# Heads of one parity form a quad: k, q and v are loaded over 128 partitions, w_in over 64

## The reference

```python
def _attn_ref(q, k, v, p):
    scale = 1.0 / np.sqrt(q.shape[-1])
    def sm_attn(qq, kk, vv):
        s = scale * np.matmul(qq, kk.transpose(0, 1, 3, 2))
        ...                      # softmax over the last axis, into a
        return np.matmul(a, vv)
    p_packed = sm_attn(p, k, v)
    return sm_attn(q, p_packed, p_packed)

def reference(...):
    x = attn_out.transpose(0, 2, 1, 3).reshape(4608, 512)
    h = x @ w_in                            # 512 -> 1024
    x = layernorm(h * softmax(h)) @ w_out   # 1024 -> 512
    h = max(x @ w1, x @ w2, x @ w3)         # 512 -> 768
    return h @ w_out2                       # 768 -> 512
```

## Time and profile before

| | |
|---|---|
| median of 3 runs | 1097.89 us |
| the profiled execution | 1094.8 us |
| its span, first to last instruction | 1093.2 us |
| TensorE busy in the span | 94% |
| VectorE, ScalarE, GpSimd busy | 55%, 32%, 23% |
| loads of k, q and v | 64 transfers, 28.3 MB of 183.2 MB moved |
| mean granted TensorE clock | 0.978 of full speed |

### The profile page before, as it was taken

One profiled execution on the slowest core, in us unless ns is written; L12 is line 12 of the kernel. 1 busy time (PEld: TensorE's weight loads), 2 busy tenths in 40 slices (PEclk: granted clock), 3 DMA queues, 4 the chain that ended last, 5 costly groups with the idle time before them and its releaser, 6 DMA issues.

```text
span 1093.2 us, 15814 instructions
## 1 busy us (share of the span) xinstructions
PE 1030.2 (94%) x6498; PEld 815.8 (75%) x6498; DVE 606.3 (55%) x980; ACT 345.6 (32%) x551; POOL 250.8 (23%) x222
## 2 busy tenths in 40 slices
PE   5778868799999999999999999999999999999998
PEld 4444534487888888888888888888888888888887
DVE  1367757767657747765646653667355563654021
ACT  3345544333423414432422233222322142222111
POOL 0112354448398439832000000000000000000000
PEclk9789989899999999999999999999999999999999
DMA  9988985234366145511575444554455535543251
GB/s 201 247 214 205 250 216 148 100 138 156 118 233 227 65 156 179 223 44 77 212 279 188 176 166 162 183 179 179 154 186 176 185 137 191 177 156 112 98 171 39
DMA packets 47144, 183.23 MB, mean 168 GB/s; under 512 B 8032, under 2 KB 8032, under 8 KB 37472
## 3 DMA queue, kind: packets, MB, share of 16 engines
q1 hardware_dynamic: 40848, 147.21, 42.6%
q0 software_dynamic: 6224, 35.00, 8.7%
HBM read 134.62 MB, written 47.58 MB: 167 GB/s over the span
## 4 chain that ended last, share of the span: by engine, by line
PE 78%; DVE 9%; DMA 5%; issue 4%; ACT 2%; POOL 1%; SPq 1%; ACTq 0%
PE ps L1088 27%; PE ps L723 24%; PE ps L1120 13%; PE ps L1111 4%; PE ps L737 2%; PE ps L988 2%; DMA q_raw<-in_q_dram 2%; PE ps L870 2%; DMA w_in_s<-in_moe_w_in_dram 2%; DVE a2T L1570 1%; DMA k_raw<-in_k_dram 1%; DVE h_lo L1479 1%; DVE spot L1776 1%; PE ps L828 1%; DVE spot L1767 1%
## 5 line engine op out<-in xcount | busy, mean ns | idle before, releaser
L1088 PE MATMUL ps<-ys,slot 128*128 128x512 f32 x1512 | 345.8, 390 | 0.5
L1088 PEld LDWEIGHTS ps<-ys,slot 128*128 128x128 f32 x1512 | 283.3, 188 | 62.4 <-ACT spot L1163 3.9
L1767 DVE TENSOR_TENSOR spot<-ps,spot 128x512 f32<-128x512 f32 x108 | 74.3, 688 | 99.7 <-PE ps L1088 74.2
L1163 ACT ACTIVATE spot<-ps 128x512 f32<-128x512 f32 x90 | 52.8, 596 | 207.5 <-PE ps L1088 196.4
L723 PE MATMUL ps<-ln_hi,w_out_s_lo 128*128 128x512 f32 x280 | 109.1, 390 | 0.0
L723 PE MATMUL ps<-ln_hi,w_out_s_hi 128*128 128x512 f32 x280 | 109.0, 389 | 0.0
L723 PE MATMUL ps<-ln_lo,w_out_s_hi 128*128 128x512 f32 x280 | 109.0, 389 | 0.0
L1120 PE MATMUL ps<-w_out_s_lo,h_hi 128*128 128x512 f32 x216 | 84.1, 389 | 0.0
L1120 PE MATMUL ps<-w_out_s_hi,h_lo 128*128 128x512 f32 x216 | 84.1, 389 | 0.0
L1120 PE MATMUL ps<-w_out_s_hi,h_hi 128*128 128x512 f32 x216 | 84.1, 389 | 0.0
L1294 ACT ACTIVATE u<-ps,neg_max 128x1024 f32<-128x1024 f32 x36 | 40.2, 1117 | 124.0 <-DVE neg_max L1645 124.0
(11 more groups left out here) (152 smaller groups left out, 1500.9 us busy)
## 6 DMA issues: line engine op xcount, KB each, us to landing
slot<-w_operands SPq DMA_DIRECT2D x36, 1792.0 KB, 7.3
w_operands<-stage POOLq DMA_DIRECT2D x18, 1024.0 KB, 4.9
k_raw<-in_k_dram SPq DMA_DIRECT2D x32, 288.0 KB, 5.9
v_raw<-in_v_dram SPq DMA_DIRECT2D x16, 576.0 KB, 9.4
q_raw<-in_q_dram SPq DMA_DIRECT2D x16, 576.0 KB
y_features<-yst SPq DMA_DIRECT2D x9, 1024.0 KB, 4.4
y_raw<-y_features SPq DMA_DIRECT2D x9, 1024.0 KB, 5.6
out_dram<-spot SPq DMA_DIRECT2D x36, 256.0 KB, 2.1
```

The source lines that it names most:

```text
L1088: last = pe.matmul(ps[:, group_bank(g, k), :], w[:, a - 1, i, kk, :], ys[:, b, j, kk, :], start=n < 4 and kk == 0 and e == 0, stop=kk == K ...
L1163: return act.activation(dst, src, ACT.Copy)
L1767: dve.tensor_tensor(dst[:, :], a, b, op).then_inc(ready, 1)
```

## The change

A quad is now the heads of one parity: quad g holds the heads g, g + 2, g + 4, g + 6. The view of k, q and v merges quad and partition: partition 64g + p reads at p x 2304 bytes behind the start of head g, which for one pair of heads is one run of neighbouring rows over all 128 partitions. So k comes in two transfers a batch (576 KB each), v and q in one each (1152 KB). The rows of w_in that belong to the heads of a quad are no longer 128 neighbours: `w_in_s` is filled by four transfers of 512 KB, each over 64 partitions and two blocks. `p` and its tile stay as they were; `scores1` picks other columns of the transposed p (`small`). The counts that TensorE waits for change with the number of transfers. Engine instructions are the same in number and shape.

```diff
-    w_in_v = w_in.rearrange("(k p) n -> p k n", p=P)
+    w_in_v = w_in.rearrange("(x l g d) n -> l d g x n", l=2, g=QUADS, d=D)
...
     def rows(t):
-        return t.rearrange("b (g h) (p j) d -> b g p h (j d)", g=QUADS, j=J)
+        return t.rearrange("b (h g) (p j) d -> b (g p) h (j d)", g=QUADS, j=J)
...
                 for x in range(2):
-                    for g in range(QUADS):
-                        sp.dma_start(k_raw[half(g), 2 * x:2 * x + 2, :, :].rearrange("p h j d -> p h (j d)"),
-                                     k_v[b, g][:, 2 * x:2 * x + 2, :]).then_inc(k_loaded[x], 16)
+                    at = slice(2 * x, 2 * x + 2)
+                    sp.dma_start(k_raw[:, at, :, :].rearrange("p h j d -> p h (j d)"), k_v[b][:, at, :])\
+                        .then_inc(k_loaded[x], 16)
...
-                for g in range(QUADS):
-                    sp.dma_start(v_raw[half(g), :, :, :].rearrange("p h j d -> p h (j d)"), v_v[b, g])\
-                        .then_inc(v_loaded, 16)
+                sp.dma_start(v_raw[:, :, :, :].rearrange("p h j d -> p h (j d)"), v_v[b]).then_inc(v_loaded, 16)
...
-                for g in range(QUADS):
-                    sp.dma_start(q_raw[half(g), :, :, :].rearrange("p h j d -> p h (j d)"), q_v[b, g])\
-                        .then_inc(q_loaded, 16)
+                sp.dma_start(q_raw[:, :, :, :].rearrange("p h j d -> p h (j d)"), q_v[b]).then_inc(q_loaded, 16)
...
                 if b == 0:
-                    sp.dma_start(w_in_s[:, :, :], w_in_v).then_inc(w_in_loaded, 16)
+                    for l in range(2):
+                        for g in range(QUADS):
+                            sp.dma_start(w_in_s[half(l), 2 * g:2 * g + 2, :], w_in_v[l][:, g]).then_inc(w_in_loaded, 16)
...
                 def small(jj, h):
-                    return pT[jj * D:(jj + 1) * D, g, h * NPACK:(h + 1) * NPACK]
+                    n = QUADS * h + g
+                    return pT[jj * D:(jj + 1) * D, n // QH, n % QH * NPACK:(n % QH + 1) * NPACK]
```

More of the change, by code:

```diff
@@ L761, in turn_k @@
                 if j % 2 == 0:
-                    pe.wait_ge(k_loaded[min(j // 2, 1)], 32 * b + 32)
+                    pe.wait_ge(k_loaded[min(j // 2, 1)], 16 * b + 16)
                 turn_rows(bank, k_raw, j).then_inc(kT_filled, 1)
@@ L815, in turn_q @@
                 if j == 0:
-                    pe.wait_ge(q_loaded, 32 * b + 32)
+                    pe.wait_ge(q_loaded, 16 * b + 16)
                 turn_rows(bank, q_raw, j).then_inc(qT_filled, 1)
             def pack(b):
-                pe.wait_ge(v_loaded, 32 * b + 32)
+                pe.wait_ge(v_loaded, 16 * b + 16)
                 pe.wait_ge(a1T_first, 2 * b + 2)
@@ L856, in merge @@
                 if b == 0:
-                    pe.wait_ge(w_in_loaded, 16)
+                    pe.wait_ge(w_in_loaded, 64)
                 if b == B - 1:
```

## The result

| | before | after |
|---|---|---|
| median | 1098.22 us (4 runs, 1094.13 to 1101.03) | 1079.72 us (4 runs, 1078.86 to 1080.79) |
| profiled execution | 1094.8 us | 1078.86 us |
| its span | 1093.2 us | 1077.1 us |

The ratio after to before is 0.9835, 95% interval 0.9802 to 0.9868: 18.5 us or 1.7% less by the medians, 15.9 us between the two profiled executions. The change is faster, by 1.3 to 2.0% in the interval.

What follows compares the result with a forecast made beforehand. TensorE was taken to bound the kernel at 78%, with most load time hidden; 3 + 0 + 3.5 + 1.5 + 0.8 + 2 = 10.8 us off gave 1084 from the profiled execution, 1087 from the median, said as 1085, 8-in-10 range 1073 to 1094.

Steps and rivals of the forecast that it cites:

- a wait for w_in above 4 us: Sign named beforehand: TensorE waiting longer than this for w_in in the profile after would show the prediction wrong.
- Step 1: Start of the kernel, first loads of k and those of batch 1: 3 us saved, bounds 1.5 to 4.
- Step 2: Load of w_in, needed at the merge of batch 0: no change, bounds -1.5 to +2 us.
- The rival "slower": At the merge of batch 0, w_in's four slices land so late that the gain is lost: 1100 us, chance 0.04.
- Step 3: Load of q for batch 5: 3.5 us less wait, bounds 1.8 and 4.2, and 1.5 us of clock behind it.
- Step 4: Load of q for batch 7: 0.8 us of TensorE's wait saved, bounds 0 and 1.8.
- Step 5: TensorE's "issue" waits in pack and scores2, read as code fetches partly queueing behind data: 2 us saved, bounds -1 and 8.
- The rival "more than the sum": Attention stage: fetches (8), w_in's wait (1.5) and clock (another 4) gain beyond the forecast: 1073 us, chance 0.17.

Runs made afterwards that it cites:

- The second experiment: The changed kernel with as many transfers of k, q and v as before, each over 128 partitions: 1081.17 us, ratio 0.9829 to the kernel before.
- the first: The changed kernel with loads of k, q and v cut back into 64-partition halves, w_in still in slices: 1100.2 us, ratio 1.002 to the kernel before.

## Why the prediction was right, and where it was off

The direction and the range (1073 to 1094) held, and so did the main reason, the rate of the loads; the gain came out larger than the 1085 said, by 5 us, and than the sum of 10.8, by 5.1 between the profiled executions (15.9). That it came this near is in part luck. Two terms were too small by about 6 us each (the waits without a releaser and the clock), and w_in, put at nothing, took 4.9 us and hid most of one of them. Of the signs named beforehand, "a wait for w_in above 4 us" was to be one of being wrong, and it came, with 7.0; the wait for q of batch 5 stayed at 2.26 us, not below one; and the dense layers start at 247 and not 251 us.

**The transfers** were read rightly. 380 GB/s was taken for rows of 2304 bytes over 128 partitions, which no row of before showed; 388, 367 and 381 were measured. The second experiment shows that the number and the size of the transfers do not matter, and the first that the gain is gone, and the order of the rows worth nothing, once each load spans 64 partitions.

**Step 1, the start**: 3 us said, 2.9 measured (18.13 to 15.20). Also the way there: ScalarE's table load and copies set the pace of the second half (its transposes wait 1.18 us for a copy now, not for data).

**Step 2, w_in**: nothing said, bounds -1.5 to +2; measured 4.9 us more wait, and 8.0 us by the run with w_in whole. The rate was right (215 and 218 for 224), and the landing close (46 to 47.5 said, 45.3 measured). What failed is that the need, like the release of q, "moves up by 3 us": it moved by 11.2, from 49.7 to 38.5, since the work before it lost two waits without a releaser (2.66 and 2.89 us) and ran more at the higher clock, and the landing by only 6.4. Here the step that spoke against the change was priced at zero because a gain of 3 us from step 1 was taken for all that moves the need. The rival "slower" was built on the same wait and named the right place, but it needed a rate of 93 GB/s or less, and 208 to 218 were measured.

**Step 3, q of batch 5**: 3.5 us said with bounds 1.8 and 4.2, measured 1.95 (4.21 to 2.26): near the end where both stores share the engines with it. Its chain in the profile after is 119.93 to 129.5 us, 9.6 us for 1.18 MB, when 7.4 + 2.6 was that bound. The clock came back as said: the merges behind it take 1.94 us.

**Step 4, q of batch 7**: 0.8 said, 0.78 measured.

**Step 5, waits without a releaser**: 2 us said with bounds -1 and 8, measured 8.0 (20.3 to 12.3), the far bound. The step read them as fetches of code that queue behind data, which the run with almost no loads supports: at one and the same instruction the wait is 4.72 us with loads in flight and 1.55 with almost nothing. That the packets are code is still a reading of the queue's name; no run shows it. What failed is where the gain was looked for. I looked at the two long waits. One stayed (4.94 to 4.72, with k and w_out_raw issued in front of that pack) and one shrank (4.77 to 2.98), while the pack of batch 1 even got more (0.97 to 2.55). The ones that went altogether are the middle ones: 2.66 in the pack of batch 0, 2.89 in `scores2` of batch 0 and 1.71 in the pack of batch 3, 7.3 us together. With all loads in halves they are back, at 2.11, 2.99 and 2.34 us, so they hang on the loads. The runs with one load wide take them apart only in part: with k wide 1.69, 1.70 and 1.79 us are left, with v wide 0.71 and 2.98 and no third, with q wide none of the three, while TensorE there waits longer for loads. That the faster loads were through before the fetch came is inferred.

**The term that was missing** is the clock over the whole stage. 1.5 us was said, for the one wait that the chain showed; 7.6 us less busy time was measured for the same matmuls. Most idle stretches over 2 us are followed by work at half speed, in whole or in part: before, transposes behind the wait of 2.89 us in `scores2` (1.97 us for eight against 1.09), after, the merge behind w_in's 7 us, 3.68 us against 1.94. The rival "more than the sum" had both of these, fetches 8 and clock 4 more, at a chance of 0.17, and was nearer to what happened than the forecast in its terms; only w_in, where it expected another gain, brought it back to 1080.

The Trainium skill's rule ("SBUF — State Buffer", section "Door 1: The DMA port swizzle"), that the rate of a transfer depends on how many of the 16 ports its partitions reach, was the right one to read this change by, for k, q, v and against w_in alike. The trace agrees in the rates: w_in's slices ran at 208 to 218 GB/s between 38 and 44 us, a little over the Trainium skill's 196 for 64 partitions. The ports themselves no run here shows.

**What stays open.** Why a fetch waits behind the data in flight as long as it does. In the pack of batch 2 the packet moves 1.7 to 3.0 us before TensorE goes on, in each of eight kernels (before, after, w_in early, the two with w_out_raw moved, k behind the pack, almost no loads, q wide). What varies is how long after the pack's first matmul it moves: 0.1 to 0.6 us with almost no loads, 5.1 to 5.6 with w_in early. No run separates the amount of data ahead from the queue it is in. Also open is how much of the stage the two fetch waits left in packs of batches 2 and 6 are worth.

## What to carry to other kernels

Look at the rate beside the busy share of the DMA engines: 100% busy at 220 GB/s beside 380 GB/s for another transfer is a shape that can be repaired, here by ordering the work so that one transfer spans 128 partitions. When such an edit moves the cost onto another transfer, price that one at the time when it will be needed after the change, and then issue it earlier if its buffer is free: moving w_in forward, from behind q of batch 1 to behind q of batch 0, gave another 6 us for nothing. In a stage of many short matmuls count an idle stretch of TensorE with what it does to the clock behind it, which here was nearly as much as the idle time itself (7.6 us against 8.5).

## What the runs showed of the hardware

- Loads of 2304-byte rows move at 367 to 388 GB/s over 128 partitions and at 224 to 240 over 64, with the DMA engines as busy in both cases (1.02 to 1.08).
- SP needs less time to issue the wider load of v or q: mostly 0.37 to 0.47 us for one over 128 partitions after the change, against mostly 0.63 for one over 64. Four of k over 128 partitions took 1.82 us at the start, four over 64 took 2.73. This does not hold for every transfer over 128 partitions: w_in whole took 0.61 us. I had taken 0.63 for k, q and v alike.
- At the same place of TensorE's program, with the same code, the last wait in the pack of batch 2, read as one for a fetch, lay between 1.55 us (almost no loads) and 5.74 us (only q wide) over these kernels.
